# Tiles 0 to 2 of a convolution + MLP kernel: scales from sums of |x|, four weight conversions on VectorE, accumulating DMAs, another load order

## The reference

```python
# attention-like dynamic convolution: x [4, 4096, 192], weight_gen [4, 4096, 8, 7]
w = exp(weight_gen - max over the 7 taps);  w = w / (sum over the 7 taps + 1e-9)
out[s, head, g] = sum_k w[s, head, k] * x_pad[s + k, head, g]     # 8 heads x 24 columns, causal
# MLP on the 16384 rows of out
h = out @ w_in                 # 192 x 2048
g = maximum(0.01 * h, h)
result = g @ w_out             # 2048 x 192, float32
```

## Time and profile before

| what | value |
|---|---|
| three timed runs | 1034.59, 1035.06, 1039.36 us, median 1035.06 |
| span of the profiled execution, first to last instruction | 1033.8 us |
| what lies between that span and the median | 1.3 us |
| TensorE (PE) busy | 1024.1 us, 99% |
| VectorE (DVE) busy | 945.2 us, 91% |
| ScalarE (ACT) busy | 631.1 us, 61% |
| GpSimd (POOL) busy | 545.6 us, 53% |

### The profile page before, as it was taken

How to read it: one execution, slowest core, us unless ns; L and a number is a source line. 1 busy time by engine, 2 the same in 40 slices (tenths; PEclk the granted TensorE clock), 3 DMA queues, 4 the chain that set the end, 5 groups by cost and what they waited for, 6 DMA issues and landing times.

```text
span 1033.8 us, 28952 instructions
## 1 busy us (share of the span) xinstructions
PE 1024.1 (99%) x12755; PEld 614.6 (59%) x12755; DVE 945.2 (91%) x1227; ACT 631.1 (61%) x1332; POOL 545.6 (53%) x369
## 2 busy tenths in 40 slices
PE   8999999999999999999999999999999999999998
PEld 4666566555655655655665565565565565556566
DVE  7999999999999999999999999999999999998611
ACT  6766566566556656565665565665566565566554
POOL 0004556545655665665565665565566556556543
PEclk9999999999999999999999999999999999999999
DMA  9101213112131310213211131210313102111100
GB/s 264 65 16 32 87 30 97 35 32 81 20 97 35 95 34 19 83 34 97 35 33 66 35 98 34 72 56 6 97 34 97 35 22 76 35 35 35 35 17 17
DMA packets 67445, 57.48 MB, mean 56 GB/s; under 512 B 56252, under 2 KB 60604, under 8 KB 65336
## 3 DMA queue, kind: packets, MB, share of 16 engines
q1 hardware_dynamic: 67196, 55.35, 19.1%
q10 hardware_dynamic: 124, 0.29, 0.1%
HBM read 29.34 MB, written 12.58 MB: 41 GB/s over the span
## 4 chain that ended last, share of the span: by engine, by line
PE 90%; DVE 6%; SPq 1%; DMA 1%; ACT 1%; issue 0%; POOL 0%; DVEq 0%; ACTq 0%; POOLq 0%
PE h_ps L969 43%; PE out_ps L1079 22%; PE t_ps L1079 22%; DVE conv L612 1%; DVE prod L605 1%; PE out_ps L1033 1%; DVE gl L654 1%; PE h_ps L951 1%; DMA rawD<-in_moe_w_in_dram 1%; PE out_ps L1043 1%; SPq L329 1%; DVE xs L644 0%; DVE xs L642 0%; SPq L332 0%; DVE wo L634 0%
## 5 line engine op out<-in xcount | busy, mean ns | idle before, releaser
L298 POOL TENSOR_TENSOR gl<-g,gh 128x512 f16<-128x512 f32 x360 | 543.6, 1537 | 479.7 <-ACT g L426 479.7
L424 ACT ACTIVATE gh<-h_ps 128x512 f16<-128x512 f32 x512 | 317.4, 620 | 373.8 <-PE h_ps L969 360.9
L1079 PE MATMUL t_ps<-wo,gh 64*128 64x384 f16 (+1 forms) x1984 | 386.6, 317 | 0.9 <-ACT gh L424 0.9
L1079 PE MATMUL out_ps<-wo,gh 64*128 64x384 f16 (+1 forms) x1984 | 386.6, 317 | 0.0
L969 PE MATMUL h_ps<-xT,whA 64*128 64x512 f16 x1920 | 364.3, 376 | 0.0
L426 ACT ACTIVATE g<-h_ps 128x512 f32<-128x512 f32 x512 | 321.8, 628 | 0.0
L612 DVE TENSOR_TENSOR conv<-conv,prod 128x768 f32<-128x768 f32 x186 | 277.8, 1493 | 1.1
L605 DVE TENSOR_TENSOR prod<-xbuf,taps 128x768 f32<-128x768 f32 x186 | 273.6, 1483 | 0.0
L1079 PE MATMUL t_ps<-wo,gl 64*128 64x192 f16 x1920 | 233.2, 243 | 1.4 <-DVE gl L654 1.4
L1079 PE MATMUL out_ps<-wo,gl 64*128 64x192 f16 x1920 | 233.2, 243 | 0.0
L1079 PEld LDWEIGHTS t_ps<-wo,gh 64*128 64x128 f16 x1984 | 181.3, 94 | 57.7 <-ACT gh L424 1.4
(11 more groups left out here) (99 smaller groups left out, 681.3 us busy)
## 6 DMA issues: line engine op xcount, KB each, us to landing
xbuf<-in_x_dram SPq DMA_DIRECT2D x15, 1344.0 KB, 6.0
out_dram<-stage SPq DMA_DIRECT2D x31, 384.0 KB, 2.4
taps<-in_weight_gen_dram SPq DMA_DIRECT2D x16, 224.0 KB, 5.9
xT_again<-xT SPq DMA_DIRECT2D x29, 64.0 KB, 2.1
rawO<-in_moe_w_out_dram SPq DMA_DIRECT2D x4, 384.0 KB, 10.0
rawA<-in_moe_w_in_dram SPq DMA_DIRECT2D x2, 512.0 KB, 8.4
xbuf<-in_x_dram SPq DMA_DIRECT2D x2, 384.0 KB, 6.6
rawD<-in_moe_w_in_dram SPq DMA_DIRECT2D x1, 512.0 KB, 7.3
```

The source lines that it names most:

```text
L298: nc.gpsimd.tensor_tensor(gl[:, f % RING, :], g[:, f % RING, :], gh[:, f % RING, :], ALU.subtract).then_inc(s_gl_p, 1)
L424: nc.scalar.activation(gh[:, f % RING, :], h_ps[f % GROUP][:], ACT.Prelu, scale=SHRINK, alpha=SLOPE).then_inc(s_gh, 1)
L1079: ins = nc.tensor.matmul(dst, a[rows, f % RING, j * P:(j + 1) * P], moved, start=i == 0 and k < 2 and a is gh and f == 0 and part != 1, st ...
```

## The change

It has five parts. (1) The row scales of tiles 0 and 1 come from a bound: ScalarE sums |x| over single rows and over the four rows that all windows share (`sum_rows`, `SUMS`), and VectorE adds up the window of each row (`windows`, `bound`); `SHRINK0` goes with it. (2) Four of the twelve weight high parts move to VectorE (`HI_BY_VECTOR`). (3) In tiles 1 and 2 four of the six additions of a convolution are DMAs that GpSimd issues and that add to their destination (`add_products`); VectorE keeps seven products and two additions. (4) `w_in` lands as A first half, D, A second half, and D's second copy in halves. TensorE sums the |w| sums itself, and `w_top` goes. (5) `gl` of a group in tiles 0 and 1 is one instruction; the warm-ups shrink, and TensorE takes D's products of a group in pairs.

```diff
-WARM_UP = (20, 9, 4)
+WARM_UP = (16, 4, 4)
...
+QUEUED = [("mul", k) for k in range(7)] + [("sum", 3), ("sum", 5)] + LAST
+BOUNDED = QUEUED[:7] + [("bound", 0)] + LAST[1:] + QUEUED[7:9]
+QUEUED_TILES = (1, 2)
...
+        SUMS = [(4, 7, 8), (5, 8, 9), (6, 9, 10), (3, 3, 7), (2, 2, 3), (1, 1, 2), (0, 0, 1)]
...
+        HI_BY_VECTOR = [("A", 0), ("A", 1), ("D", 1), ("O", 0)]
...
+            def add_products(t):
+                i, acc = QUEUED_TILES.index(t), conv[:].rearrange("p j d -> p (j d)")
+                pool.wait_ge(s_conv, conv_done(t, ("mul", 1)))
+                nc.gpsimd.dma_start(acc, prod[:, 0, :], accum_op=ALU.add).then_inc(s_add_first, DMA)
+                pool.wait_ge(s_conv, conv_done(t, ("mul", 3)))
+                nc.gpsimd.dma_start(prod[:, 1, :], prod[:, 2, :], accum_op=ALU.add).then_inc(s_add_next, DMA)
+                pool.wait_ge(s_conv, conv_done(t, ("mul", 5)))
+                nc.gpsimd.dma_start(prod[:, 3, :], prod[:, 4, :], accum_op=ALU.add).then_inc(s_add_last, DMA)
+                pool.wait_ge(s_add_first, DMA * (2 * i + 1))
+                pool.wait_ge(s_add_next, DMA * (i + 1))
+                nc.gpsimd.dma_start(acc, prod[:, 1, :], accum_op=ALU.add).then_inc(s_add_first, DMA)
...
-            load_last_rows(0, 0, FF, 0)
-            for half in range(2):
-                sp.dma_start(rawA[:, c], w_in[0:P, c]).then_inc(s_rawA[half], DMA)
-            load_last_rows(1, 0, PIECE, 1)
+            load_columns(0)
+            load_last_rows(sp, 0, 0, FF, 0)
+            load_columns(1)
+            load_last_rows(sp, 1, 0, FF // 2, 1)
...
+                    sp.wait_ge(s_conv, conv_done(m + 1, ("mul", K - 1)))
+                    if m == 0:
+                        sp.wait_ge(s_x_sum, 2 * N_SUMS)
                     load_chunk(c + 2, c % 2)
...
+                if n == 1:
+                    bound_second()
...
+            def sum_rows(t, k):
+                nc.scalar.activation(x_abs[:, 0:(last - first) * D],
+                                     xbuf[:, 0, (t * SUB + first) * D:(t * SUB + last) * D], ACT.Abs,
+                                     accum_out=x_rows_sum[:, t, col:col + 1]).then_inc(s_x_sum, 1)
...
+                elif what == "sum":
+                    if k == 3:
+                        dve.wait_ge(s_add_first, DMA * 2 * (i + 1))
+                        dve.wait_ge(s_add_last, DMA * (i + 1))
+                    ins = nc.vector.tensor_tensor(acc, acc, prod[:, k, :], ALU.add)
...
             def group(n):
-                for f in range(n % NG * GROUP, (n % NG + 1) * GROUP):
-                    lo_of_g(n // NG * NF + f, f)
+                dve.wait_ge(s_g, (n + 1) * GROUP)
+                nc.vector.tensor_tensor(gl[:, at, :], g[:, at, :], gh[:, at, :], ALU.subtract).then_inc(s_gl_v, GROUP)
...
+            def first_tile():
+                lo_pieces(0, 2)
+                take_transposed(0)
+                split_hi(("A", 1))
+                split_hi(("D", 1))
+                lo_pieces(2, 4)
+                for n in range(4, N_SOFTMAX):
+                    softmax0(1, n)
+                out_scale0()
+                split_hi(("O", 0))
                 lo_pieces(4, 5)
                 group(0)
                 lo_pieces(5, 7)
-                conv1(5, 9)
+                early_conv(1, ("mul", 0), ("mul", 4))
                 lo_pieces(7, 8)
-                conv1(9, 11)
+                early_conv(1, ("mul", 5), ("mul", 6))
                 group(1)
                 lo_pieces(8, 10)
-                conv1(11, N_CONV)
+                early_conv(1, ("bound", 0), ("out_scale", 0))
+                early_conv(1, ("sum", 3), ("sum", 5))
                 lo_pieces(10, 11)
-                lo_of_x(1)
                 group(2)
+                lo_of_x(1)
                 lo_pieces(11, 12)
```

More of the change, by code:

```diff
@@ L36, with conv_of, conv_before, conv_done @@
 N_CONV = len(CONV)
-SCALED = CONV.index(("scale", 0)) + 1
+LAST = [(what, 0) for what in ("top", "mask", "unscale", "scale", "out_scale")]
+QUEUED = [("mul", k) for k in range(7)] + [("sum", 3), ("sum", 5)] + LAST
+BOUNDED = QUEUED[:7] + [("bound", 0)] + LAST[1:] + QUEUED[7:9]
+QUEUED_TILES = (1, 2)
 N_SOFTMAX = 6
+def conv_of(t):
+    return BOUNDED if t == 1 else QUEUED if t in QUEUED_TILES else CONV
+def conv_before(t):
+    return sum(len(conv_of(u)) for u in range(1, t))
+def conv_done(t, op):
+    return conv_before(t) + conv_of(t).index(op) + 1
 CONV_TO = (4, 8, CONV.index(("top", 0)))
@@ L281, in load_halos, with load_last_rows @@
                                 ).then_inc(s_x0, DMA)
+        def load_last_rows(queue, half, first, last, n):
+            queue.dma_start(rawD[half * DR:(half + 1) * DR, first:last], w_in[P:D, first:last]).then_inc(s_rawD[n], DMA)
         block = ctx.enter_context(nc.Block())
@@ L392, in abs_wo @@
             def abs_wo(n):
[L394 removed]
+                first, last = ((0, 1), (1, 2), (2, 4))[n]
+                for piece in range(first, last):
+                    act.wait_ge(s_rawO[piece], DMA)
                 if n > 0:
                     act.wait_ge(s_wo_abs, n)
[L397 to L399 removed]
+                nc.scalar.activation(wo_abs[:, 0:(last - first) * PIECE_F, :], rawO[:, first * PIECE_F:last * PIECE_F, :], ACT.Abs,
+                                     accum_out=w_sum[:, 1, n:n + 1]).then_inc(s_wo_abs, 1)
             def hi_of_x(t):
                 if t == 0:
[L403 removed]
+                    act.wait_ge(s_scales0, 4)
                 else:
[L405 removed]
+                    act.wait_ge(s_conv, conv_done(t, ("sum", 5) if t == 1 else ("scale", 0)))
                     if t > BY_PE:
@@ L495, in abs_w_in, with bound_second @@
                 rows = raw.shape[0]
-                nc.scalar.activation(w_abs[0:rows, :], raw, ACT.Abs, accum_out=w_sum[0:rows, 0, n:n + 1]
+                nc.scalar.activation(w_abs[0:rows, 0:raw.shape[1]], raw, ACT.Abs, accum_out=w_sum[0:rows, 0, n:n + 1]
                                      ).then_inc(s_w_abs, 1)
+            def sum_rows(t, k):
+                col, first, last = SUMS[k]
+                if t == 0 and first < HALO:
+                    act.wait_ge(s_x0, 2 * B * DMA)
+                if k + t > 0:
+                    act.wait_ge(s_x_sum, t * N_SUMS + k)
+                nc.scalar.activation(x_abs[:, 0:(last - first) * D],
+                                     xbuf[:, 0, (t * SUB + first) * D:(t * SUB + last) * D], ACT.Abs,
+                                     accum_out=x_rows_sum[:, t, col:col + 1]).then_inc(s_x_sum, 1)
+            def bound_second():
+                act.wait_ge(s_chunk[0], DMA)
+                for k in range(N_SUMS):
+                    sum_rows(1, k)
             def exp_half(half):
@@ L510, in _ @@
             exp_half(1)
+            act.wait_ge(s_x_own, DMA)
+            for k in range(N_SUMS):
+                sum_rows(0, k)
             act.wait_ge(s_w_sum, 2)
+            act.wait_ge(s_rawA[0], DMA)
+            abs_w_in(0, rawA[:, 0:FF // 2])
             act.wait_ge(s_rawD[0], DMA)
[L513 to L520, removed]
-                abs_wo(n)
[L522 to L533, removed]
+            abs_w_in(1, rawD[0:DR, :])
+            act.wait_ge(s_rawA[1], DMA)
+            abs_w_in(2, rawA[:, FF // 2:FF])
+            hi_of_x(0)
+            take_transposed(0, 0)
+            abs_wo(0)
+            take_transposed(0, 1)
+            split_hi(("D", 0))
+            for n in range(1, 3):
+                abs_wo(n)
+            leaky(0)
             for n in range(2 * NG):
```

191 lines of the change are left out of this document (106 added, 85 removed).

## The result

| | median us | runs | lowest to highest | profiled execution, its span |
|---|---|---|---|---|
| before | 1035.21 | 5 | 1034.59 to 1039.36 | 1033.8 span |
| changed | 1042.94 | 5 | 1042.89 to 1045.08 | 1044.47, 1042.7 span |

The ratio is 1.0076, with a 95% interval of 1.0060 to 1.0093: the change costs 7.7 us. The forecast was 1032.9 us with a range up to 1037.5, so it had both the sign and the size wrong. The profiled execution is one of the two longer of the five runs, 1.5 us above the median (mean granted clock 0.995 in these two, 0.997 in the other three).

What follows compares the result with a forecast made beforehand. PE is busy 99% of the span, but VectorE's tile 0 list sets when its steady rhythm starts. 2.7 won less 0.5 stall takes 2.2 off 1033.8, so 1031.6; plus 1.3 between span and median, 1032.9 us, range 1031.0 to 1037.5.

Steps and rivals of the forecast that it cites:

- 2.7 us won in VectorE's list: Tile 0's VectorE work ends sooner, so tile 1's first PE product comes at 51.0 instead of 53.72 us.
- 0.5 of stall: VectorE's wait for tile 1's adding DMAs before its additions, about 0.5 us, taken off the gain.
- the term for meeting the load: Tile 1's fourth adding DMA meets the next rows' load; 1.0 us more charged for that one.
- d = 3.7: Duration in us taken for one adding DMA of 384 KB, bounds 2.4 and 10; threshold 4.0.
- DMAs late: Rival: tile 1's adding DMAs take 8.3 us each, stall 8.6, 1041.0 us; chance 0.2 over 2.7 us, 0.07 over 8.
- The load order leaves the end of the w_in sums where it was: Start: the new landing order costs nothing; the last accumulator is still read at 15.62 us.
- PE's clock falls: Rival: with fewer warm-ups PE runs 20 to 24 us at 1.2 GHz, 4 us half hidden, 1034.9 us; chance 0.08.
- the prices on VectorE: Start-to-start costs in tile 0's list: high parts 0.42 and 0.55 us; single gl instruction saves three starts, 2.2.
- products are not slowed: Rival judged: GpSimd issuing DMAs slows VectorE's products in tile 1, at most 4.8 us, 1037.2; chance of no gain 0.1.
- Tile 2's DMAs cost next to nothing: Tile 2's adding DMAs have some 8 us for their pair and about 2 us of slack: cost nothing.
- The bound of the gain: The win is a shift of tile 1's first PE product, 2.7 us, less a 0.5 stall: 2.2 us.
- All later tiles move with it: Any shift of tile 1's first product, at 53.72 us before, carries whole and once to all later tiles.

Runs made afterwards that it cites:

- experiment 1: Changed kernel, but the next rows' load is issued only after VectorE's last addition of tile 1: 1036.14 us, ratio 0.9997 to the kernel before.
- 2: Changed kernel with three adding DMAs, the fourth addition of tiles 1 and 2 on VectorE, load still early: 1039.08 us, ratio 1.0035.
- 11: version 8 with the next rows' load put back behind the seventh product of tile 1: 1038.92 us, ratio 1.0021.
- 6: Changed kernel with the load after tile 1's last addition and three adding DMAs, the fourth addition on VectorE: 1034.97 us, ratio 0.9999.
- version 8: Changed kernel with late load, three adding DMAs, and the old landing and sum order of w_in: 1033.77 us, ratio 0.9989; best found.
- 5: Changed kernel with the load after tile 1's last addition, and the old landing and sum order of w_in: 1034.33 us, ratio 0.9985.
- 10: Changed kernel with only the old landing and sum order of w_in; the load stays early: 1042.07 us, ratio 1.0059.
- 9: version 8, but VectorE makes O2's low part ahead of tile 1's three additions: 1034.46 us, ratio 0.9993.
- 4: Changed kernel, but VectorE makes O2's low part and gl 2 ahead of tile 1's two additions: 1041.55 us, ratio 1.0053.
- experiment 3: Changed kernel without adding DMAs, all six additions of tiles 1 and 2 on VectorE: 1045.09 us, ratio 1.0094.

## Why the prediction was wrong

Its sum was 2.7 us won in VectorE's list less 0.5 of stall, which puts tile 1's first product at 51.5. It came at 61.8. The 10.3 us between them are these.

- **The step that failed: the adding DMAs of tile 1.** The stall was 6.3 instead of 0.5: **5.8 us**. The larger part is the term for meeting the load. I charged 1.0 us to the fourth DMA; by experiment 1 it is 8.62 - 4.1 = 4.5, which makes 3.5 of the 5.8. The third DMA met the load as well (8.7 us), and I charged it nothing; experiments 2 and 11 show what that costs when the fourth is gone. The rest of the 5.8, some 2.3, is there without any load. The duration taken for one DMA, d = 3.7, was too low (4.87 for the second, 4.1 for the fourth), and the 0.54 us from the one's landing to the other's issue was not in the sum. With these the stall is 38.24 + 4.87 + 0.54 + 4.1 less 45.95, where VectorE asks, or 1.8 us; experiment 1 has 1.76. I had the right comparison in hand, `rawO`'s 384 KB that took 10.0 under crowding, and used it as the rival's price, not as that of the DMAs beside a load. The rival *DMAs late* has the right place and mechanism, and its 1041.0 is the nearest of all the figures. It let every DMA take 8.3, where only the third and the fourth do.
- **The clock behind the stall was left out.** I priced idle time of PE at its length. After 5.98 us of it, PE's next 32 products took 5.21 us instead of 2.81: **2.4 us** more.
- **The start was late, for two reasons: 2.1 us.** "The load order leaves the end of the w_in sums where it was" was wrong: they ended at 17.1 instead of 15.8, 1.3 us late. Experiments 6 and 8 give 1.2 for the order alone, 1 and 5 give 0.9 to 1.3, the changed kernel and 10 give 1.8 to 2.0. The other 1.1 us are the clock from 16 to 24 us (0.91 and 0.67), against which 0.3 us were won on the way from the sums to PE (4.1 us at full clock, forecast 4.4). That is the rival *PE's clock falls*, at its place and with about half its price; it came in this one profile and in none of the ten experiments (1.00 in each from 20 to 24 us), so it may be missing from the median. PE started at 22.3, not 20.2, and the whole list of VectorE runs some 2.1 to 2.4 us late from there (the fourth product ends near 38.0, not 35.6). These three terms add up to 10.3.
- **Right:** the prices on VectorE. A high part takes 0.49 and 0.61 us by itself, about 0.4 start to start (taken 0.42 and 0.55); one `gl` 2.28 (2.2); products are not slowed. The first projection lies 9.3 us behind PE's first product (31.64 - 22.30; forecast 29.4 - 20.2 = 9.2, before 12.53). No clock of 0.62 at 28 to 32 us is left. Tile 2's DMAs cost next to nothing (0.45 us of waiting).
- **The bound of the gain was right as well.** With both failures taken away (version 8) the mark comes at 51.52 and the gain there is 2.2 us, of which 1.6 shows in the span (1032.2 against 1033.8) and 1.3 in the median. "All later tiles move with it" holds to within 0.8 us: what follows the mark takes 980.1 us before and 980.9 in the changed kernel. The time outside the span is 1.8 to 1.9 us in every run of either kernel that lists both, where I took 1.3 from a span and a median of different executions.

The Trainium skill (DMA: Bandwidth & Descriptors, Anatomy of one DMA) has a fit for DMAs issued by GpSimd from which 384 KB are an estimate of 2.9 us. The traces here do not agree for a DMA that adds: 3.9 to 5.3 us with no load in flight, and 8.6 to 9.4 beside one. Whether the adding, or the other adding DMAs that overlap with each, make the difference was not tried.

## What to carry to other kernels

Price a DMA that something waits for at its duration beside whatever transfer will be in flight, not at its duration alone, and look for a large load that the same progress counter releases: here both hung on VectorE's products, and however early the list ran, they met. The price goes on every waited-for transfer that is still in flight then, also on one issued shortly before the load. Moving the load behind the wait cost nothing here, because nothing needed it soon. And a stall in front of TensorE is to be priced above its length: here 3.3 us and more of waiting put part or all of the next 32 products at the 1.2 GHz level.

## What the runs showed of the hardware that was not expected

- **An adding DMA beside a load.** 384 KB within on-chip memory take 4.0 to 5.2 us from issue to landing in tile 1 with no load in flight (experiments 1, 5, 6, 8, 9; another adding DMA overlaps with each). Beside a 1344 KB load from memory the third, sent 0.6 us ahead of it, takes 8.7, 8.7, 9.4, 9.3 and 9.1 (changed, 2, 4, 10, 11), and the fourth, sent 2 us after it, 8.6, 9.3 and 9.2 (changed, 4, 10). The load itself takes 7.9 to 9.4 us there, 5.5 to 5.7 when it comes later, and 5.6 when it comes early with no adding DMA beside it (experiment 3).
- **The clock after idle time.** For the 32 projection products after a wait of PE: wait 0.84, 1.40, 1.70 us, then 2.81 us; 3.30, 3.65, 3.75 us, then 4.47, 4.23, 5.30; 5.98 and 6.50 us, then 5.21 and 5.14. In each case with the longer time the granted clock of the 4 us stretch with most of these products was 0.50 to 0.66.
- **Landing of loads scatters.** With the same order of loads, the last of the three `w_in` pieces landed between 15.0 and 16.9 us in the six profiles with the new order, and between 13.4 and 14.4 in the five with the old one. PE's first product followed the last sum by 4.1 us in ten of the eleven and by 5.2 in the one with the lower clock.
